# The first pair of heads: halves, split straight from PSUM, operand rows written by engines; coefficients made in the third pair

## The reference

```python
q_bits = (np.einsum('bhsd,dk->bhsk', q, proj) > 0).astype(np.int64)   # and k_bits
mask = q_bucket[:, :, :, None] == k_bucket[:, :, None, :]
scores = scale * np.matmul(q, k.transpose(0, 1, 3, 2))                # scale = 1/8
scores = np.where(mask, scores, -1000000000.0)
attn = np.exp(scores - max) / (sum + 1e-09);  out = np.matmul(attn, v)
# second stage: h = x @ w_in; g = P(h) / (Q(h) + 1e-6), P from a[0..3], Q from |b|; g @ w_out
# third stage: gate, argmax, relu(xe @ w1[e]) @ w2[e], times the gate's weight
```

## Time and profile before

| what | us |
|---|---|
| median of 3 runs | 840.25 |
| the profiled execution | 838.99 |
| its span | 837.1 |
| TensorE busy | 778.8 (93%) |
| VectorE, ScalarE, POOL busy | 564.3, 488.8, 455.0 |
| scores of tile 0 start | 23.70 |
| exponential of tile 0 starts | 32.61 |

### The profile page before, as it was taken

One profiled execution on the slowest core, in us unless ns is written; L12 is line 12 of the kernel. 1 busy time (PEld: TensorE's weight loads), 2 busy tenths in 40 slices (PEclk: granted clock), 3 DMA queues, 4 the chain that ended last, 5 costly groups with the idle time before them and its releaser, 6 DMA issues.

```text
span 837.1 us, 13297 instructions
## 1 busy us (share of the span) xinstructions
PE 778.8 (93%) x4246; PEld 689.3 (82%) x4246; DVE 564.3 (67%) x962; ACT 488.8 (58%) x971; POOL 455.0 (54%) x402
## 2 busy tenths in 40 slices
PE   3599999999999889999999999995899999999995
PEld 3489899898898779999999999885788888888883
DVE  3278788788898588787878787885444454454441
ACT  2277788788799798878778777764123224223000
POOL 2231643652645497557657644425895669756700
PEclk9599999999999999999999999997899999999998
DMA  7698878878662590690493004055752627461200
GB/s 167 132 207 191 181 169 190 185 171 203 135 194 62 167 308 1 223 295 0 154 353 126 1 20 182 1 189 189 227 193 73 239 94 245 141 226 26 83 14 19
DMA packets 72387, 125.01 MB, mean 149 GB/s; under 512 B 33438, under 2 KB 36094, under 8 KB 68224
## 3 DMA queue, kind: packets, MB, share of 16 engines
q1 hardware_dynamic: 64816, 92.28, 41.6%
q10 hardware_dynamic: 5024, 25.56, 9.0%
q0 software_dynamic: 2480, 6.31, 2.0%
HBM read 60.26 MB, written 34.24 MB: 113 GB/s over the span
## 4 chain that ended last, share of the span: by engine, by line
PE 85%; ACT 4%; DVE 3%; POOL 2%; issue 2%; DMA 2%; SPq 1%; ACTq 0%; POOLq 0%
PE ps L1326 7%; PE ps L1415 5%; PE ps L1416 5%; PE ps L1414 5%; PE ps L1400 5%; PE ps L1398 5%; PE ps L1399 5%; PE ps L1560 4%; PE ps L1584 4%; PE ps L1586 4%; PE ps L1585 4%; PE ps L1561 4%; PE ps L1562 4%; PE ps L1316 4%; PE ps L1317 4%; PE ps L1338 4%
## 5 line engine op out<-in xcount | busy, mean ns | idle before, releaser
L763 POOL TENSOR_TENSOR split<-wraw,split 128x512 f32 (+1 forms) x112 | 140.3, 1289 | 53.6 <-ACT split L909 50.7
L909 ACT ACTIVATE split<-wraw 128x512 f32 (+1 forms) x128 | 68.8, 617 | 141.3 <-PE ps L1562 65.9
L1057 DVE TENSOR_TENSOR ptl<-ps,pth 128x512 fp32r<-128x512 f32 x144 | 98.7, 685 | 36.0 <-ACT pth L847 34.0
L740 POOL TENSOR_TENSOR hw<-hw,ha 128x384 f32<-128x384 f32 x64 | 65.2, 1018 | 75.8 <-ACT hw L921 75.8
L847 ACT ACTIVATE pth<-ps 128x512 fp32r<-128x512 f32 x144 | 86.6, 602 | 31.4 <-PE ps L1326 31.2
L1037 DVE TENSOR_REDUCE negmax<-ps 128x1 f32<-128x768 f32 x96 | 91.0, 948 | 14.8 <-PE ps L1317 14.8
L1326 PE MATMUL ps<-cst,pr 128*128 128x128 f32 x576 | 88.5, 274 | 1.1 <-ACT pr L838 1.1
L838 ACT ACTIVATE pr<-ps,negmax 128x768 f32<-128x768 f32 x96 | 86.8, 904 | 3.2 <-DVE negmax L1037 3.2
L1398 PE MATMUL ps<-xh,wih 128*128 128x384 f32 x256 | 86.3, 337 | 2.0 <-DVE hp L1091 2.0
L1400 PE MATMUL ps<-xh,wil 128*128 128x384 f32 x256 | 86.1, 336 | 0.0
L1399 PE MATMUL ps<-xl,wih 128*128 128x384 f32 x256 | 85.8, 335 | 0.0
(11 more groups left out here) (195 smaller groups left out, 1981.2 us busy)
## 6 DMA issues: line engine op xcount, KB each, us to landing
routed<-blank SPq DMA_DIRECT2D x33, 771.0 KB, 14.8
wraw<-in_moe_w ACTq DMA_DIRECT2D x24, 1024.0 KB, 5.5
wraw<-in_moe_w SPq DMA_DIRECT2D x8, 1024.0 KB, 5.7
operand<-qk_hi SPq DMA_DIRECT2D x16, 384.0 KB, 4.5
operand<-qk_lo SPq DMA_DIRECT2D x32, 192.0 KB, 4.2
operand<-qk_hi SPq DMA_DIRECT2D x32, 192.0 KB, 4.5
operand<-mask SPq DMA_DIRECT2D x16, 384.0 KB, 4.7
xg<-routed SPq DMA_DIRECT2D x19, 256.0 KB
```

The costliest lines, as they stand in the source:

```text
L763: pool.tensor_tensor(split_piece(E_LO[x], ring, k), wraw[:, x, i, :], split_piece(E_HI[x], ring, k).bitcast(F32), ALU.subtract).then_inc(e ...
L1057: dve.tensor_tensor(ptl[:, at:at + CW], ps[:, 4 + c % 2, :], pth[:, at:at + CW].bitcast(F32), ALU.subtract).then_inc(ptl_done, 1)
```

## The change

The start-up of pair 0 is rewritten.

- q and k are loaded in two halves (three of six blocks of 128 positions each), with a semaphore for each half; ScalarE issues four loads, SyncE four. proj is loaded by POOL's queue.
- `first_split`: ScalarE writes the upper part straight from PSUM, VectorE the lower part from PSUM and the upper part. There are no raw tiles and no POOL split for pair 0; POOL's semaphore `qk_split` counts from pair 1 on.
- Head 0's own rows are written by engines: planes 0 and 1 by POOL, 2 and 3 by ScalarE. Three transfers (`first_rows`) bring its other rows. Head 1 keeps its five row transfers.
- `first_mask`: VectorE writes the masks of both heads into the operands, 64 partitions at a time; five pieces ahead of slot 0, three (head 1's) behind the maxima of slots 0, 2 and 4. For this the words of `sel` stand in swapped halves, and for the later pairs the mask transfer reads the rows that it writes.
- TensorE: the signs of the first half are compared before the lower part of the second half is projected; the comparisons use banks 7, 6, 4, 5.
- `coefficients` is called at slot 48 (the third pair).
- `op_landed` gives the counts of the operand transfers, which differ for pair 0.

```diff
+        FIRST_SEL = (7, 6, 4, 5)
+        def op_landed(p, o):
+            return 96 * (p // 2 + 1) - (0 if p % 2 else (48, 16)[o])
 # SyncE
+            def first_rows():
+                op, hi, lo = operands[0][0], qk_hi[0], qk_lo[0]
+                sp.wait_ge(first_lo, 1)
+                sp.dma_start(op[D:P, 0, 0:HALF].bitcast(F32), lo[0:D, 0, 0:HALF].bitcast(F32)).then_inc(s_op[0][0], 16)
+                sp.wait_ge(first_hi, 4)
+                sp.dma_start(op[D:P, 2, :].bitcast(F32), hi[0:D, 1, :].bitcast(F32)).then_inc(s_op[0][0], 16)
+                sp.wait_ge(first_lo, 3)
+                sp.dma_start(op[D:P, 0, HALF:S].bitcast(F32), lo[0:D, 0, HALF:S].bitcast(F32)).then_inc(s_op[0][0], 16)
-            for o in range(2):
-                sp.dma_start(nat[0][:, 0, :, o, :], q_h[o, :, :, :]).then_inc(s_qk[0], 16)
-            sp.dma_start(pr_raw[0:D, :], proj).then_inc(s_proj, 16)
-            sp.dma_start(pr_raw[D:P, :], proj).then_inc(s_proj, 16)
+            for ts, landed in ((slice(0, HT), s_half), (slice(HT, NT), s_qk[0])):
+                for o in range(2):
+                    sp.dma_start(nat[0][:, 0, ts, o, :], q_h[o, :, ts, :]).then_inc(landed, 16)
...
             load_qk(1)
+            first_rows()
             load_v(0)
-            for o in range(2):
-                operand_rows(0, o)
-                mask_rows(0, o)
+            operand_rows(0, 1)
 # POOL
-            split_qk(0, 0)
+            for o in range(2):
+                pool.dma_start(pr_raw[o * D:(o + 1) * D, :], proj).then_inc(s_proj, 16)
+            pool.wait_ge(first_hi, 3)
+            pool.tensor_copy(operands[0][0][0:D, 0:2, :], qk_hi[0][0:D, 0:1, :].bitcast(F32).broadcast_to([D, 2, S])).then_inc(first_own, 1)
             split_v(0)
 # ScalarE
+            def first_split(half):
+                for x in range(2):
+                    act.wait_ge(first_pe, 2 * half + x + 1)
+                    act.activation(qk_hi[0][:, x, half * HALF:(half + 1) * HALF], ps[:, 2 * half + x, 0:HALF], ACT.Copy, scale=(0.125, 1.0)[x]).then_inc(first_hi, 1)
+            first_split(0)
             act.wait_ge(s_proj, 32)
...
+            first_split(1)
             act.wait_ge(s_const, 32)
             act.activation(sel[:, :], csel[:, :], ACT.Copy).then_inc(sel_made, 1)
+            act.wait_ge(first_hi, 4)
+            act.activation(operands[0][0][0:D, 2, :], qk_hi[0][0:D, 1, :].bitcast(F32), ACT.Copy).then_inc(first_own, 1)
+            act.wait_ge(first_lo, 4)
+            act.activation(operands[0][0][0:D, 3, :], qk_lo[0][0:D, 1, :].bitcast(F32), ACT.Copy).then_inc(first_own, 1)
...
             for s in range(NSLOT + 1):
+                if s == 2 * PAIR_SLOTS:
+                    coefficients()
 # VectorE
+            def first_split(half):
+                for x in range(2):
+                    k, c = 2 * half + x, slice(half * HALF, (half + 1) * HALF)
+                    dve.wait_ge(first_hi, k + 1)
+                    dve.scalar_tensor_tensor(out=qk_lo[0][:, x, c], in0=ps[:, k, 0:HALF], scalar=(0.125, 1.0)[x], in1=qk_hi[0][:, x, c].bitcast(F32), op0=ALU.mult, op1=ALU.subtract).then_inc(first_lo, 1)
+            first_split(0)
...                                   # proj's lower parts (L998 to L1001) as before
+            first_split(1)
+            def first_mask(half, x, o):
+                c, other = slice(half * HALF, (half + 1) * HALF), slice((1 - o) * D, (2 - o) * D)
+                bank, row = ps[other, FIRST_SEL[2 * half + x], 0:HALF], operands[0][o][other, 2 * x + 1, c]
+                dve.wait_ge(first_pe, 6 + 3 * half + x)
...                                   # the two tensor_scalar of L1007 and L1009, from bank to row
+            first_mask(0, 0, 0)
+            first_mask(0, 0, 1)
+            first_mask(0, 1, 0)
+            first_mask(1, 0, 0)
+            first_mask(1, 1, 0)
...
+                if s in (0, 2, 4):
+                    first_mask(*((0, 1, 1), (1, 0, 1), (1, 1, 1))[s // 2])
 # TensorE
+            pe.wait_ge(proj_lo, 4)
+            first_proj_hi(0)
+            first_proj_lo(0)
+            first_proj_hi(1)
             pe.wait_ge(sel_made, 1)
+            first_sel(0)
+            first_proj_lo(1)
+            first_sel(1)
 # scores
+                if g == 0:
+                    pe.wait_ge(first_own, 3)
+                    pe.wait_ge(first_dve, 5)
+                if g == NT:
+                    pe.wait_ge(first_dve, 8)
```

More of the change, by code:

```diff
@@ L544, in mask_rows @@
             def mask_rows(p, o):
[L546 to L551, removed]
+                sp.wait_ge(prep_out, prep_no(p, 9) + 1)
+                other = slice((1 - o) * D, (2 - o) * D)
+                sp.dma_start(operands[p % 2][o][other, 1:4:2, :].bitcast(F32), mask[other, 0:2, :].bitcast(F32)).then_inc(s_op[p % 2][o], 16)
+            def first_rows():
[6 more added lines that the diff above has]
+                sp.dma_start(op[D:P, 0, HALF:S].bitcast(F32), lo[0:D, 0, HALF:S].bitcast(F32)).then_inc(s_op[0][0], 16)
             def inverse_out(p):
@@ L794, in _ @@
         def _(act):
[L795 to L799, removed]
+            for ts, landed in ((slice(0, HT), s_half), (slice(HT, NT), s_qk[0])):
+                for o in range(2):
+                    act.dma_start(nat[0][:, 1, ts, o, :], k_h[o, :, ts, :]).then_inc(landed, 16)
+            def first_split(half):
[3 more added lines that the diff above has]
+            first_split(0)
             act.wait_ge(s_proj, 32)
@@ L1001, in _ @@
                 dve.tensor_tensor(wproj[rows, x // 2 * 2 + 1, cols], pr_raw[rows, :], wproj[rows, x // 2 * 2, cols].bitcast(F32), ALU.subtract).then_inc(proj_lo, 1)
[L1002 to L1009, removed]
+            first_split(1)
[3 more added lines that the diff above has]
+                dve.wait_ge(first_pe, 6 + 3 * half + x)
+                if x == 0:
+                    dve.tensor_scalar(row, bank, NBITS - 0.5, BIG, ALU.is_ge, ALU.mult).then_inc(first_dve, 1)
+                else:
+                    dve.tensor_scalar(row, bank, -float(NBITS), -1.0, ALU.add, ALU.max).then_inc(first_dve, 1)
+            first_mask(0, 0, 0)
[3 more added lines that the diff above has]
+            first_mask(1, 1, 0)
             def step(p, k):
@@ L1286, in step @@
                     pe.wait_ge(proj_lo, 4)
-                    pe.wait_ge(qk_split, 4 * p - 2 + 2 * half + 2)
+                    pe.wait_ge(qk_split, 4 * p - 4 + 2 * half + 2)
                     hi, lo = qk_hi[p % 2], qk_lo[p % 2]
@@ L1322, in turn @@
                 wait(pe, ptl_done, c - 1)
+                if c == 0:
+                    pe.wait_ge(first_dve, 8)
                 for x, (u, kt, t) in enumerate(chunk_blocks(c)):
@@ L1345, in _, with first_proj_hi, first_proj_lo, first_sel @@
                 mm.then_inc(first_pe, 1)
-            pe.wait_ge(proj_lo, 4)
-            for half in range(2):
-                c, bank = slice(half * HALF, (half + 1) * HALF), ps[:, 4 + half, 0:HALF]
[L1349 to L1358, removed]
+            def first_proj_hi(half):
+                pe.wait_ge(first_hi, 2 * half + 2)
+                for x in range(4):
+                    pe.matmul(ps[:, 4 + half, 0:HALF], wproj[:, x, :], qk_hi[0][:, x // 2, half * HALF:(half + 1) * HALF], start=(x == 0), stop=False)
+            def first_proj_lo(half):
+                c, bank = slice(half * HALF, (half + 1) * HALF), ps[:, 4 + half, 0:HALF]
+                pe.wait_ge(first_lo, 2 * half + 2)
                 pe.matmul(bank, wproj[:, 0, :], qk_lo[0][:, 0, c], start=False, stop=False)
                 pe.matmul(bank, wproj[:, 2, :], qk_lo[0][:, 1, c], start=False, stop=True).then_inc(first_pe, 1)
+            def first_sel(half):
+                pe.wait_ge(first_act, half + 1)
+                for x in range(2):
+                    pe.matmul(ps[:, FIRST_SEL[2 * half + x], 0:HALF], sel[:, x * P:(x + 1) * P], bits[:, half, :], start=True, stop=True).then_inc(first_pe, 1)
+            pe.wait_ge(proj_lo, 4)
+            first_proj_hi(0)
+            first_proj_lo(0)
+            first_proj_hi(1)
             pe.wait_ge(sel_made, 1)
[L1362 to L1365, removed]
+            first_sel(0)
+            first_proj_lo(1)
+            first_sel(1)
             for s in range(NSLOT):
```

49 lines of the change are left out of this document (21 added, 28 removed).

## The result

The changed kernel takes 827.13 us (median of 4 runs, 826.13 to 828.33) against 840.06 for the kernel before; the ratio is 0.985, with a 95% interval of 0.983 to 0.987. That is 12.9 us less. The forecast was 825.0 with a range of 821 to 831, and within it an own range of 822.5 to 827; rival 1 stood at 827.5. The profiled execution took 826.13, its span 824.3 (before 837.1), so 12.8 less.

The account below looks back on a forecast made before the run. TensorE is busy 93% of the span, but a chain of start-up waits delays the attention. Gains of 7.15, 6.2 and 2.5, less 0.2 for masks and 0.35 for rows, leave 15.3 us: 825.0, range 821 to 831.

Parts of the forecast that it names:

- rival 1: Start-up: the clock doesn't stay up between projection and first rounds; gain 12.8 us, 827.5, chance 0.18.
- Term C: First rounds up to scores(4): TensorE's clock rises at 13 to 14 and stays, gaining 2.5 us (bounds 0 and 2.9).
- The collision on VectorE: Start-up: VectorE's fourth subtraction for proj may wait for POOL's copy, costing 0 to 1.5 us, taken as 0.5.
- Term A: Start-up to scores(0): starts at 16.05 instead of 23.70, 7.65 us earlier, taken as 7.15 (bounds 8.4 to 4.2).
- the halves' later landing: Loads of q and k: first half lands at 4.9 (bounds 4.2 and 6.65), first transpose at 5.0.
- late rows of head 0: Ahead of scores(0): row transfers may land 0 to 0.7 us behind 16.05, taken as 0.35.
- Term B: First exponential: follows scores(0) by 2.7 us instead of 8.9, gaining 6.2.
- Late masks: First rounds: three masks behind maxima on VectorE delay a raw copy and the next maximum by 0 to 0.6, taken as 0.2.
- Coefficients at slot 48: Third pair: two activations of 0.2 us moved there on ScalarE cost 0 to 0.4, taken as 0.
- proj by POOL: Start-up: proj loaded by POOL's queue lands between 4.6 and 10, taken as 7.0, costing 0; the late end costs 3.
- That all of it arrives at the end: After scores(4): the old order row for row, 15 to 16 us earlier, with the gain kept to the end.

Follow-up runs that it names:

- e10: Changed kernel plus transposes of the identity that nobody reads, where TensorE is idle in the start-up: 824.70 us, ratio 0.982.
- e3: Changed kernel with POOL's copy of head 0's own rows waiting until VectorE has made proj's four lower parts: 824.92 us.
- e2: Kernel before with one edit, the coefficients made at slot 48: 833.27 us, ratio 0.9925.
- e1: Changed kernel with the coefficients made ahead of slot 0 again: 829.15 us.
- e7: Changed kernel with proj loaded by SyncE behind q again, instead of by POOL: 827.50 us, ratio 0.9846.
- e12: Kernel before plus 8 filler matmuls in TensorE's pause in the second stage: 837.19 us against 839.83, ratio 0.9976.
- e11: Changed kernel with POOL's copy later, one head 1 mask later, 8 filler matmuls in the second stage and idle start-up transposes: 822.30 us, ratio 0.9786.
- e5: Changed kernel plus 8 filler matmuls into an unread bank in TensorE's pause in the second stage: 825.38 us.

## Why the prediction was right, and where its steps were off

**Term C, and the level of the clock, is the least certain step.** I said that the clock "should rise at 13 to 14 and stay". In the first profile it rose between 14.2 and 14.8 (projection matmuls of 0.69 and then 0.34), fell at 18.1 and was back at 21.5; in two others it never rose before 25.6. The reason given, "no pause over 0.7 us before the scores", did not fit my own walk, which has the last comparison at 14.45 and scores(0) at 16.05 behind two masks. The trace has pauses of 0.67 and 1.06 there. Forecast and rival 1 are executions of one kernel: scores(0) to the first exponential 2.07 and 2.73, the last exponential 14.9 and 12.5 earlier than before. The median, 827.13, lies just outside the forecast's own range (822.5 to 827) and 0.4 from rival 1 (827.5), so the usual execution is nearer to the rival that got a chance of 0.18 than to the forecast with 0.57. That the time still fell well inside 821 to 831 is owed to a range that held both. The Trainium skill ("TensorE: Matmul & The Clock Gate", section "HAM oscillation — how this bites in real kernels") tells of kernels whose waits between bursts of matmuls bring the low level back again and again. The traces agree in kind, with shorter waits: the level fell behind the short waits of the start-up and behind the 2.95 us at 288, but in some executions and not in others. I had weighed it too low. The 2.4 us of e10 are what filling the idle of the start-up was worth in the median.

**The collision on VectorE was mis-sized.** Term A counted 0.5 of a possible 1.5, with the fourth subtraction at risk. Nearly all of it came: the fourth began at 8.93, POOL's copy at 8.91, 0.02 earlier, and it lasted 1.46. e3 takes that out. This is most of why scores(0) came at 17.32 and not at 16.05 to 16.55; the halves' later landing (first transpose at 5.51, not 5.0) is the other part. Term A measured 6.4 instead of 7.15. From the projection's start to scores(0) it was 6.87 (7.25 counted). TensorE's wait there ended with VectorE's mask, so the 0.35 counted for late rows of head 0 came to nothing.

**Term B held**: the first exponential stands 2.07 behind scores(0) and had stood 8.9. B and C together, by scores(4), were 14.3-6.4 = 7.9 of 8.7 counted. e2 gave 6.8 for B alone in the median (6.2 counted; in its profile the first exponential is 6.4 earlier, the rest is the clock's). e1 gave only 2.2 in the new order. Both fit, as B's part is a wait for SyncE's list, which the new order shortens by itself: there the coefficients land at 22.2 instead of 32.4.

**Late masks**: TensorE's first turn of blocks waited 0.38 for VectorE's third late mask (25.09 in place of 24.7), within the 0 to 0.6 of the step. **Coefficients at slot 48**: from tile 14 (58.59) to tile 44 (133.25) the distance to before is 14.87 to 14.91, and no table load stands at the two activations (81.35 and 81.44), so they cost nothing. **proj by POOL**: nothing, as counted (e7).

**That all of it arrives at the end** failed by 2.1 us in the profile: the clock fell in the pause of the second stage, and it had not in the profile of before. By e12 the kernel before has that loss as well in many executions, so in the medians it should largely cancel; there the start-up's clock is the likelier cause of the missing 2.4 (15.3 forecast, 12.9 measured), as in two of three profiles the last exponential is only 12.5 and 12.9 earlier. That split of the medians is argued, not measured. The step was unsound in one respect: I took one profiled execution's tail as the kernel's.

**What stays open**: how often each fall happens; that would need many profiles. And in e11's profile the clock was low for 24 us around the routing between second and third stage, 17 in that of before and in the changed kernel's first; what that costs I didn't separate.

## What to carry to other kernels

A start-up is a chain over all queues: the largest single gain here was two tiny activations behind a late 1 KB transfer in a strictly ordered list, and their price shrank as the other parts got faster, so measure such edits alone and together. Before adding work to POOL, look which VectorE instructions with two SBUF operands run at that moment; here one wait on the POOL side took 1.3 us off VectorE's four subtractions. Where TensorE pauses a few us ahead of dense work, cheap matmuls into an unread bank can pay: 1.6 and some 2 us in the median here. The spread stayed as it was (3.1 in e5, 4.0 in e12); only the idle transposes of the start-up came with a smaller one (1.6 in e10), and with the other edits (e11) it was 4.0 again. And one profile is one execution: where its clock falls, take a second before naming a cause.

## What the runs showed of the hardware that I had not expected

The same kernel's start-up ran at two clock patterns in two executions, 2.4 us apart at the end of the attention, which the device times alone (826.13 and 828.97) don't tell from a loss elsewhere. The clock column reads 1.00 before the first change in the trace, even where matmuls of 384 columns last 0.52; their length is the safer witness. Loads of 96 KB in the start-up landed in 3.3 to 3.7 us (medians) against 4.0 for k's of 192 KB: little shorter each, yet the first transposes start 1.3 to 1.6 earlier (5.51 against 6.79 and 7.07).
